# A scan-and-feed-forward kernel: ScalarE copies the first block's updates into the states instead of VectorE's additions

## The chip, the core and the metric

The kernel runs on one core of one Trainium2 chip. The metric is the device time of one execution in microseconds; the time of a kernel is the median of several executions. Engine names are those of the profile: PE is TensorE (its matmuls; PEld its weight loads), DVE is VectorE, ACT is ScalarE, POOL is GpSimd, SP is SyncE, which only issues transfers here.

## The reference

A gated linear attention over 768 positions is followed by two feed-forward layers over 3072 tokens of width 384, with 2048 hidden units each:

```
state = 0                                  # [4 batches, 8 heads, 48, 48]
for t in range(768):
    state = alpha[t][:, None] * state + outer(k[t], v[t])
    y[t]  = q[t] @ state
x = y as [3072 tokens, 384]
x = mish(x @ w_in) @ w_out                 # mish(h) = h * tanh(softplus(h))
out = (x' @ w2_in) -> h ; (h * cos(h)) @ w2_out
```

All of it is float32.

## The kernel before, in words

**The attention in chunks.** The sequence is cut into 6 blocks of 128 positions. A chunk c is one block of one batch: c = 4 * block + batch, so there are 24 chunks, and chunks 0 to 3 are the first block. For each chunk, a scan over the decays (`shrink`, line 713, into `suffix`) gives what is left of each key at the end of the chunk, and a second scan (`grow`, line 724, into `growth`) scales the queries. The products keys by suffix (`keys`) and queries by growth (`queries`) are made by VectorE for the first chunks and by GpSimd (lines 929 and 936) from chunk 4 on. TensorE turns the scaled keys (`turn`, line 370), multiplies keys by queries (`scores`, lines 394 and 387), and VectorE multiplies the scores by a triangle of ones and zeros (`mask`, line 746 or 752, into `probs`). TensorE then multiplies `probs` by the values (`values`, lines 434 and 439), adds what the state gives (line 453), and forms the chunk's update of the state: keys by values, in PSUM.

**The state.** `state` in SBUF holds, for each of the 4 batches, 4 pairs of heads, 96 rows (48 for each head of a pair, at partitions 0 and 64) and 96 columns. Only the blocks where a head meets itself may be non-zero; ScalarE sets the whole buffer to zero at the start (line 681, semaphore `state_zero`). The four updates of the first block lie in PSUM banks 3 and 4, two in each. `add_state(c)` (line 787) adds update c to the zeroed state of its batch, in two instructions of 48x192, one for each head of the pairs. Each counts up `sum_ready`. From chunk 4 on GpSimd first decays the state (`decay_state`, line 943, which wants `sum_ready` at 2 for chunk 4), and the two halves of a chunk are added by `add_first` (line 769) and `add_second` (line 778).

**The feed-forward layers in tiles.** 16 pieces of the weights and 6 blocks of tokens give 96 tiles per layer. A step s issues the first product of tile s (`first_product`, line 496, 9 matmuls of 128x512) and the second product of tile s - 3 (`second_product`, line 519, also 9). Float32 is split into a high and a low part: ScalarE makes the high part of a weight piece (line 573), and VectorE or GpSimd subtracts it from the raw piece to get the low part (`split_w`: line 800 on VectorE for pieces 1 and 3 of the first layer, line 914 on GpSimd for pieces 0, 2 and 4 to 15). ScalarE computes mish (line 619) and the high part of its result (line 612), GpSimd the low part (`g_rest`, line 922).

**The order around the change.** Each engine has one list of work written out by hand and runs it in that order; semaphores tie the lists together. TensorE runs chunks 0 to 3, then steps 0, 1, 2 ... In step 2 it also does `turn(4)` and `scores(4)`; in step 3 the first product of tile 3, then the update of chunk 4 (`halves_update`, line 413), `values(4)` and the second product of tile 0; in step 5 `turn(5)` and `scores(5)`; in step 7 `turn(6)`, the update of chunk 5, `scores(6)`, `values(5)`. `halves_update(4)` waits for the masks of chunk 4 (`probs_ready`), for all eight additions to the states (`sum_ready`) and for the turned keys; tile 3's first product waits for piece 3's low part from VectorE; `scores(c)` waits for the keys and queries of chunk c, and `scores(5)` for `add_second(4)` too. VectorE's list reads: low part of piece 1, `shrink(4)`, `grow(4)`, `add_state(0)`, low part of piece 3; then in step 1 `clear_probs` (line 759, which zeroes a quarter of `probs`) and `add_state(1)` to `add_state(3)`; in step 2 the masks of chunk 4; in step 3 `add_first(4)`, `shrink(5)`, `grow(5)`, `keep_x_lo(4)` (line 793), `add_second(4)`; in step 4 `shrink(6)`, `grow(6)`; in step 5 the masks of chunk 5. GpSimd's list reads: `keys(4)`, `queries(4)`, `decay_state(4)`, then low parts of mish and of weights in turn (tile 0, piece 4, tile 1, piece 5, tile 2, piece 6), `keys(5)`, `queries(5)`, `decay_state(5)`, tile 3, piece 7, `keys(6)`, `queries(6)`. ScalarE ends its start with the high part of piece 3 and goes on with mish of tile 0.

Of the kernel before, what the change touches and what calls it, by code (L numbers as in the profile page):

```python
# [8 lines left out]
ALU = mybir.AluOpType  # L9
ACT = mybir.ActivationFunctionType  # L10

BATCH, HEADS, SEQ, D = 4, 8, 768, 48
# [4 lines left out]
PAIRS = HEADS // 2  # L17
# [25 lines left out]
def values_at(s):  # L43

    n = s + FT - 3
    if s >= 3 and n % PER_CHUNK == 0 and n // PER_CHUNK < CHUNKS:
        return n // PER_CHUNK
    return None


def scores_at(s):

    return {2: BATCH, 5: BATCH + 1}.get(s)
# [54 lines left out]
def program(nc, aqk_in, v_in, w_in, mid, out):  # L108
    with ExitStack() as ctx:
        def sb(name, shape, dt=F32):  # L110
            return ctx.enter_context(nc.sbuf_tensor(name, shape, dt))

        def sem(name):
            return ctx.enter_context(nc.semaphore(name))
# [29 lines left out]
        state = sb("state", [P, BATCH, PAIRS, 2 * D])  # L144
# [42 lines left out]
        def update_of(c, half=None):  # L187

            if c < BATCH:
                return banks[3 + c // 2][:, c % 2 * PAIRS * D:(c % 2 + 1) * PAIRS * D]  # L190
            return (banks[1][:, 0:PAIRS * D], banks[6][:, P * 2:P * 2 + PAIRS * D])[half]
# [6 lines left out]
        state_zero = sem("state_zero")  # L198
# [18 lines left out]
        upd_done = sem("upd_done")  # L217
        sum_ready = sem("sum_ready")
# [22 lines left out]
        def alive(tile):  # L241
            return 0 <= tile < 2 * TILES
# [325 lines left out]
        def _(act):  # L568
            def split_w(piece):
                act.wait_ge(w_in_sem[piece % RAWS], 16 * (piece // RAWS + 1))  # L570
                if piece >= FT:
                    act.wait_ge(out_done, TILES - FT + piece - FT + 1)
                nc.scalar.activation(w_hi[:, piece % FT, :], w_raw[:, piece % RAWS, :], ACT.Copy).then_inc(whi_ready, 1)  # L573
# [8 lines left out]
            def keep_x_hi(c):  # L582
                j, b = c // BATCH, c % BATCH
                act.wait_ge(y_done, c + 1)
                if j >= 2 and b == 0:
                    act.wait_ge(h_done, FT * (j - 1))
                nc.scalar.activation(x_hi[:, j % 2, :, b * P:(b + 1) * P],
                                     turn_bank(c)[:, 0:DM].rearrange("p (k t) -> p k t", k=KT),
                                     ACT.Copy).then_inc(xhi_ready, 1)

            def split_x2(j, k):
                if k == 0:
                    act.wait_ge(x2_in, 16 * (j - BLOCKS + 1))
                    act.wait_ge(h_done, FT * (j - 1))
                nc.scalar.activation(x_hi[:, j % 2, k, :], x_raw[:, k, :], ACT.Copy).then_inc(xhi_ready, 1)
# [45 lines left out]
            def step(s):  # L641
                if alive(s - 1) and s - 1 < TILES:
                    g_part(s - 1)
                c = values_at(s)
                if c is not None and c > BATCH:
                    if next_scores(c) is not None:
                        keep_keys(next_scores(c))
                    keep_x_hi(c)
                if alive(s):
                    if s < TILES:  # L650
                        mish(s)
                    else:
                        turns(s)
                if s == 2 * TILES:
                    fold(s - 1)
                if alive(s - 2) and s - 2 >= TILES:
                    g_part(s - 2)
                if alive(s - 1) and s - 1 >= TILES:
                    if s < 2 * TILES:
                        fold(s - 1)  # L660
                    cosine(s - 1)
                if s % FT == LAG - 1 and s > FT:
                    take_acc(s // FT - 1)
                piece = split_at(s)
                if piece is not None:
                    split_w(piece)
                if scores_at(s) is not None:
                    keep_keys(scores_at(s))
                if values_at(s) == BATCH:
                    keep_x_hi(BATCH)  # L670
                jk = x2_split(s)
                if jk is not None:
                    split_x2(*jk)
# [24 lines left out]
            split_w(2)  # L698
            keep_x_hi(3)
            split_w(3)  # L700
            for s in range(STEPS):
                step(s)

        @block.vector
        def _(dve):
# [50 lines left out]
            def clear_probs():  # L756

                dve.wait_ge(y_done, BATCH)
                nc.vector.memset(probs[0:HALF, :, :, HALF:P], 0.0).then_inc(probs_zero, 1)
# [18 lines left out]
                    nc.vector.tensor_tensor(state[rows, c % BATCH, :, cols], update_of(c, 1)[rows, :].rearrange(  # L778
                        "d (p e) -> d p e", p=PAIRS), mid_state[rows, :, cols], ALU.add).then_inc(sum_ready, 1)

            def add_state(c):
                dve.wait_ge(upd_done, BATCH)
                dve.wait_ge(state_zero, 1)
                for i in range(2):
                    rows = slice(64 * i, 64 * i + D)
                    here = state[rows, c % BATCH, :, D * i:D * i + D]
                    nc.vector.tensor_tensor(here, update_of(c)[rows, :].rearrange("d (p e) -> d p e", p=PAIRS),
                                            here, ALU.add).then_inc(sum_ready, 1)

            def keep_x_lo(c):  # L790
                j, b = c // BATCH, c % BATCH
                dve.wait_ge(xhi_ready, c + 1)
                nc.vector.tensor_tensor(x_lo[:, j % 2, :, b * P:(b + 1) * P],
                                        turn_bank(c)[:, 0:DM].rearrange("p (k t) -> p k t", k=KT),
                                        x_hi[:, j % 2, :, b * P:(b + 1) * P].bitcast(F32),
                                        ALU.subtract).then_inc(xlo_ready, 1)

            def split_w(piece):
                dve.wait_ge(whi_ready, piece + 1)
                nc.vector.tensor_tensor(w_lo[:, piece % FT, :], w_raw[:, piece % RAWS, :],  # L800
                                        w_hi[:, piece % FT, :].bitcast(F32),
                                        ALU.subtract).then_inc(wlo_ready[1], 1)
# [15 lines left out]
            def reduce_angle(tile):  # L818
                n = tile - TILES
                part = banks[7]  # L820
                un, tn, h = u[:, tile % 2, :], t[:, tile % 3, :], h_of(tile)
                dve.wait_ge(u_ready, n + 1)
                nc.vector.tensor_scalar(un, un, ROUND, ROUND, ALU.add, ALU.subtract).then_inc(um_ready, 1)  # L823
                dve.wait_ge(um_ready, n + 1)
                nc.vector.scalar_tensor_tensor(part, un, -C1, h, ALU.mult, ALU.add).then_inc(rr_ready, 1)
                dve.wait_ge(rr_ready, n + 1)
                nc.vector.scalar_tensor_tensor(tn, un, -C2, part, ALU.mult, ALU.add).then_inc(w_ready, 1)  # L827
# [8 lines left out]
            def step(s):  # L836
                if alive(s) and s >= TILES:
                    reduce_angle(s)
                if alive(s - 1) and s - 1 >= TILES:
                    gate(s - 1)  # L840
                if s % FT == LAG - 1 and s > FT:
                    take_acc(s // FT - 1)
                if s == 1:
                    clear_probs()
                    for c in range(1, BATCH):
                        add_state(c)
                if scores_at(s) is not None:
                    mask(scores_at(s))
                c = values_at(s)
                if c is not None:  # L850
                    add_first(c)
                    if c == BATCH:
                        shrink(c + 1)
                        grow(c + 1)
                    keep_x_lo(c)
                    if next_scores(c) is not None:
                        mask(next_scores(c))
                    if c < UPDATES:
                        add_second(c)
                piece = split_at(s)  # L860
                if piece is not None and lo_owner(piece) == 1:
                    split_w(piece)
                c = prepared_at(s)
                if c is not None and c > BATCH + 1:
                    shrink(c)
                    grow(c)
                jk = x2_split(s)
                if jk is not None:
                    split_x2(*jk)
# [32 lines left out]
            split_w(1)  # L902
            shrink(4)
            grow(4)
            add_state(0)
            split_w(3)
            for s in range(STEPS):
                step(s)

# [118 lines left out]
```

## Time and profile before

| | us |
|---|---|
| median of 3 executions | 888.18 |
| the three executions | 887.71, 888.18, 893.39 |
| the profiled execution, device time | 889.28 |
| its span in the profile | 887.5 |
| TensorE busy | 876.0 (99%) |
| VectorE, ScalarE, GpSimd busy | 418.4, 411.1, 372.2 |
| mean granted TensorE clock | 0.998 of full |

The span is the time from the first to the last instruction that the profile shows; the device time of the same execution holds 1.78 us more. The rest of the document names times from the start of the span. A row such as "[0.96 <-DVE w_lo L800]" says that the engine sat idle for 0.96 us before the instruction, until VectorE's instruction of line 800 was done.

### The profile page before, as it was taken

The numbers are of one execution on the slowest core, as the hardware profiler recorded it, in microseconds if no ns is written. First come the engines' busy times: TensorE is split into PE (matmuls) and PEld (weight loads), VectorE is DVE, ScalarE is ACT, GpSimd is POOL, SyncE is SP. The second block draws the span as 40 slices with busy tenths as digits, with TensorE's granted clock in tenths as the row PEclk, the third lists the DMA queues.
The fourth block names the chain that finished last, engine by engine and source line by source line (L and its number), as shares of the span: only waits on it lengthen the run. The fifth ranks groups of instructions, "written<-read, shape, count | busy, mean of one in ns | idle before, by whom it ended". The sixth has DMA issues, their size and how long they took to land.

```text
span 887.5 us, 16403 instructions
## 1 busy us (share of the span) xinstructions
PE 876.0 (99%) x6686; PEld 727.4 (82%) x6686; DVE 418.4 (47%) x660; ACT 411.1 (46%) x707; POOL 372.2 (42%) x287
## 2 busy tenths in 40 slices
PE   8899999999999999999999999999999999999998
PEld 7688888888888888888888788888888888888886
DVE  8864322233332222230022766666565666666564
ACT  4444332232333233322455756565565656565554
POOL 3788654444345443432355433323232333323232
PEclk9999999999999999999999999999999999999999
DMA  9635321113212111210133200200200200200000
GB/s 223 191 105 150 88 75 39 40 41 87 64 44 75 39 41 40 75 31 1 54 124 108 72 1 1 71 1 1 72 0 1 72 1 0 72 1 1 37 0 36
DMA packets 17163, 48.28 MB, mean 54 GB/s; under 512 B 2752, under 2 KB 2752, under 8 KB 17088
## 3 DMA queue, kind: packets, MB, share of 16 engines
q1 hardware_dynamic: 17088, 47.23, 18.4%
q8 instruction: 53, 0.87, 0.4%
q14 instruction: 22, 0.18, 0.1%
HBM read 37.79 MB, written 9.44 MB: 53 GB/s over the span
## 4 chain that ended last, share of the span: by engine, by line
PE 94%; DVE 3%; issue 1%; ACT 1%; DMA 0%; POOL 0%; ACTq 0%; DVEq 0%; POOLq 0%
PE low L519 44%; PE low L496 33%; PE pair L496 11%; PE top L453 2%; PE top L434 1%; PE top L439 1%; PE pair L387 1%; PE low L413 1%; PE low L370 1%; DVE growth L724 1%; DVE suffix L713 0%; DMA shared<-aqk_in 0%; DVE w_lo L800 0%; DVE probs L746 0%; ACT w_hi L573 0%
## 5 line engine op out<-in xcount | busy, mean ns | idle before, releaser
L922 POOL TENSOR_TENSOR g_lo<-g,g_hi 128x512 fp32r<-128x512 f32 x192 | 260.9, 1359 | 471.2 <-ACT g_hi L612 471.2
L519 PE MATMUL low<-g_hi,w_hi 128*128 128x512 f32 x576 | 224.6, 390 | 0.3 <-DVE x_out L816 0.3
L519 PE MATMUL low<-g_hi,w_lo 128*128 128x512 f32 x576 | 224.1, 389 | 0.0
L612 ACT ACTIVATE g_hi<-g 128x512 fp32r<-128x512 f32 x192 | 120.6, 628 | 117.7 <-PE low L519 116.9
L519 PE MATMUL low<-g_lo,w_hi 128*128 128x512 f32 x576 | 165.7, 389 | 0.0
L519 PEld LDWEIGHTS low<-g_hi,w_hi 128*128 128x128 f32 x576 | 108.1, 188 | 23.8 <-DVE x_out L816 0.7
L519 PEld LDWEIGHTS low<-g_lo,w_hi 128*128 128x128 f32 x576 | 108.1, 188 | 22.6
L519 PEld LDWEIGHTS low<-g_hi,w_lo 128*128 128x128 f32 x576 | 108.1, 188 | 22.4
L496 PE MATMUL low<-x_hi,w_hi 128*128 128x512 f32 x432 | 124.0, 395 | 1.4 <-DVE w_lo L800 1.0
L496 PE MATMUL low<-x_lo,w_hi 128*128 128x512 f32 x432 | 121.6, 390 | 0.0
L496 PE MATMUL low<-x_hi,w_lo 128*128 128x512 f32 x432 | 121.5, 390 | 0.0
L619 ACT ACTIVATE g<-low 128x512 f32<-128x512 f32 x96 | 57.5, 599 | 135.9 <-PE low L496 135.9
L823 DVE TENSOR_SCALAR shared<-shared 128x512 f32<-128x512 f32 x96 | 42.2, 440 | 138.1 <-ACT shared L626 138.1
L496 PEld LDWEIGHTS low<-x_hi,w_lo 128*128 128x128 f32 x432 | 81.1, 188 | 17.3
L496 PEld LDWEIGHTS low<-x_lo,w_hi 128*128 128x128 f32 x432 | 81.1, 188 | 17.1
L496 PEld LDWEIGHTS low<-x_hi,w_hi 128*128 128x128 f32 x432 | 79.4, 188 | 19.0 <-issue 1.6
L769 DVE TENSOR_TENSOR mid_state<-low,state 48x192 f32<-48x192 f32 x40 | 14.2, 355 | 164.6 <-PE pair L413 124.5
L827 DVE SCALAR_TENSOR_TENSOR shared<-shared,top 128x512 f32<-128x512 f32 x96 | 65.9, 686 | 3.3
L626 ACT ACTIVATE shared<-low 128x512 f32<-128x512 f32 x48 | 28.7, 598 | 79.8 <-PE low L496 79.8
L626 ACT ACTIVATE shared<-pair 128x512 f32<-128x512 f32 x48 | 28.7, 598 | 74.2 <-PE pair L496 74.2
L639 ACT ACTIVATE shared<-shared 128x512 f32<-128x512 f32 x96 | 60.8, 633 | 3.0
L633 ACT ACTIVATE shared<-shared 128x512 f32<-128x512 f32 x96 | 59.8, 623 | 0.2 <-DVE shared L827 0.2
(107 smaller groups left out, 924.3 us busy)
## 6 DMA issues: line engine op xcount, KB each, us to landing
w_raw<-w_in SPq DMA_DIRECT2D x32, 384.0 KB, 3.1
shared<-aqk_in SPq DMA_DIRECT2D x44, 192.0 KB, 3.7
v_sb<-v_in SPq DMA_DIRECT2D x24, 256.0 KB, 4.4
shared<-aqk_in SPq DMA_DIRECT2D x48, 96.8 KB, 3.8
mid<-x_out SPq DMA_DIRECT2D x6, 768.0 KB, 5.3
shared<-mid SPq DMA_DIRECT2D x6, 768.0 KB, 5.8
out<-x_out SPq DMA_DIRECT2D x5, 768.0 KB, 4.1
out<-x_out SPq DMA_DIRECT2D x3, 256.0 KB, 2.4
```

The costliest lines, as they stand in the source:

```text
L453: mm = nc.tensor.matmul(turn[32 * n:32 * n + 32, k * P + t:k * P + t + HALF], ahead[0:ROWS, p, cols], q_of(c)[0:ROWS, p, t:t + HALF], star ...
L496: mm = nc.tensor.matmul(bank, wp[:, f, k * P:(k + 1) * P], xp[:, j % 2, k, :], start=(n == 0), stop=(n == 3 * KT - 1))
L519: mm = nc.tensor.matmul(acc[m], wp[:, f, DM + m * P:DM + (m + 1) * P], gp[:, tile % GB, :], start=(f == 0 and n == 0), stop=(f == FT - 1 a ...
L612: nc.scalar.activation(g_hi[:, tile % GB, :], g[:, tile % GB, :], ACT.Copy).then_inc(ghi_ready, 1)
L619: nc.scalar.activation(g[:, tile % GB, :], h_of(tile), ACT.Mish).then_inc(g_ready, 1)
L626: nc.scalar.activation(u[:, tile % 2, :], h_of(tile), ACT.Identity, scale=1.0 / TWO_PI).then_inc(u_ready, 1)
L633: nc.scalar.activation(here, here, ACT.Abs).then_inc(abs_ready, 1)
L639: nc.scalar.activation(here, here, ACT.Sin, scale=-1.0, bias=TWO_PI / 4).then_inc(r_ready, 1)
L769: nc.vector.tensor_tensor(mid_state[rows, :, cols], update_of(c, 0)[rows, :].rearrange("d (p e) -> d p e", p=PAIRS), state[rows, c % BATCH ...
L823: nc.vector.tensor_scalar(un, un, ROUND, ROUND, ALU.add, ALU.subtract).then_inc(um_ready, 1)
L827: nc.vector.scalar_tensor_tensor(tn, un, -C2, part, ALU.mult, ALU.add).then_inc(w_ready, 1)
L922: nc.gpsimd.tensor_tensor(g_lo[:, tile % GB, :], g[:, tile % GB, :], g_hi[:, tile % GB, :].bitcast(F32), ALU.subtract).then_inc(glo_ready, 1)
```

## The change

ScalarE gets a function `start_state(c)`, called for the four batches at the end of its start, between the high part of piece 3 and step 0. It copies the update of batch c out of PSUM into the zeroed state, in two ACTIVATE instructions of 48x192, after the zeroing of the state is done and after both updates of the PSUM bank are there. VectorE's `add_state` is gone, both the call for batch 0 before the low part of piece 3 and the three calls in step 1. `clear_probs` moves from step 1 to the place behind the low part of piece 3. The counts of `sum_ready` are the same.

```diff
--- before
+++ after
@@ scalar
+            def start_state(c):
+
+                act.wait_ge(state_zero, 1)
+                act.wait_ge(upd_done, c // 2 * 2 + 2)
+                for i in range(2):
+                    rows = slice(64 * i, 64 * i + D)
+                    nc.scalar.activation(state[rows, c, :, D * i:D * i + D], update_of(c)[rows, :].rearrange(
+                        "d (p e) -> d p e", p=PAIRS), ACT.Copy).then_inc(sum_ready, 1)
+
...
             split_w(2)
             keep_x_hi(3)
             split_w(3)
+            for c in range(BATCH):
+                start_state(c)
             for s in range(STEPS):
                 step(s)
@@ vector
-            def add_state(c):
-                dve.wait_ge(upd_done, BATCH)
-                dve.wait_ge(state_zero, 1)
-                for i in range(2):
-                    rows = slice(64 * i, 64 * i + D)
-                    here = state[rows, c % BATCH, :, D * i:D * i + D]
-                    nc.vector.tensor_tensor(here, update_of(c)[rows, :].rearrange("d (p e) -> d p e", p=PAIRS),
-                                            here, ALU.add).then_inc(sum_ready, 1)
...
-                if s == 1:
-                    clear_probs()
-                    for c in range(1, BATCH):
-                        add_state(c)
                 if scores_at(s) is not None:
                     mask(scores_at(s))
...
             shrink(4)
             grow(4)
-            add_state(0)
             split_w(3)
+            clear_probs()
             for s in range(STEPS):
                 step(s)
```

## Rows read from the trace of the kernel before

**Rows 1.** The page, busy time of each engine, its share of the span and instructions.

```profile
PE 876.0 (99%) x6686; PEld 727.4 (82%) x6686; DVE 418.4 (47%) x660; ACT 411.1 (46%) x707; POOL 372.2 (42%) x287
```

**Rows 2.** Waits of TensorE from 40 us on: us in total, times, longest.

```profile
PE low L413 <- DVE probs L752: 2.0, 1, 2.0
...
PE low L519 <- DVE x_out L816: 0.3, 1, 0.3
```

**Rows 3.** Timeline of TensorE: start us, us, what [idle before, releaser].

```profile
34.08 0.69 PE L387 MATMUL pair<-shared 48*64 48x64 f32 x32
...
35.73 0.94 PE L496 MATMUL low<-x_hi,w_hi 128*128 128x512 f32 x3 [0.96 <-DVE w_lo L800]
...
40.03 0.25 PE L413 MATMUL low<-v_sb,kd_t 64*48 64x48 f32 x2 [1.99 <-DVE probs L752]
...
43.76 0.50 PE L519 MATMUL low<-g_hi,w_hi 128*128 128x512 f32 x1
```

**Rows 4.** Windows: each engine's busy us, TensorE's granted clock, DMA share, GB/s.

```profile
40.03:43.83 3.80, 3.80 (x113) 3.41 (x113) 3.03 (x3) 0.00 (x0) 3.80 (x3) 0.55 0.50 151
...
59.90:62.64 2.74, 2.74 (x146) 2.58 (x145) 0.71 (x2) 0.84 (x2) 2.74 (x3) 1.00 0.16 33
```

**Rows 5.** Timeline of VectorE from 30 to 74 us.

```profile
30.47 2.17 DVE L724 TENSOR_TENSOR_SCAN growth<-shared,first_inv 112x516 f32<-112x516 f32 x1
...
33.32 2.27 DVE L800 TENSOR_TENSOR w_lo<-w_raw,w_hi 128x768 fp32r<-128x768 f32 x1
...
35.64 0.48 DVE L759 MEMSET probs<- 64x512 f32 x1
...
36.15 2.29 DVE L787 TENSOR_TENSOR state<-low,state 48x192 f32<-48x192 f32 x6
...
38.47 1.41 DVE L752 TENSOR_TENSOR probs<-pair,causal 64x512 f32<-64x512 f32 x2
...
41.51 4.12 DVE L713 TENSOR_TENSOR_SCAN suffix<-shared,first_one 112x516 f32<-112x516 f32 x1
...
55.27 1.41 DVE L752 TENSOR_TENSOR probs<-pair,causal 64x512 f32<-64x512 f32 x2
...
70.80 2.58 DVE L724 TENSOR_TENSOR_SCAN growth<-shared,first_inv 112x516 f32<-112x516 f32 x1
```

**Rows 6.** Line 800 on VectorE, durations in ns, min/median/max.

```profile
L800 DVE TENSOR_TENSOR w_lo<-w_raw,w_hi x10: 947/958/2268, 27.2 to 504.3; 128x768 fp32r<-128x768 f32 x10
```

**Rows 7.** Timeline of GpSimd from 32 to 75 us.

```profile
32.79 1.19 POOL L936 TENSOR_TENSOR shared<-shared,growth 112x512 f32<-112x512 f32 x1 [1.23 <-DVE growth L724]
...
33.93 0.83 POOL L943 TENSOR_TENSOR state<-state,suffix 112x384 f32<-112x384 f32 x1
...
41.48 1.27 POOL L922 TENSOR_TENSOR g_lo<-g,g_hi 128x512 fp32r<-128x512 f32 x1
...
48.19 1.19 POOL L936 TENSOR_TENSOR shared<-shared,growth 112x512 f32<-112x512 f32 x1 [1.23 <-DVE growth L724]
...
56.18 1.19 POOL L936 TENSOR_TENSOR shared<-shared,growth 112x512 f32<-112x512 f32 x1
...
72.25 2.12 POOL L929 TENSOR_TENSOR shared<-shared,suffix 112x512 f32<-112x512 f32 x1
```

**Rows 8.** Timeline of ScalarE from 26 to 33 us.

```profile
26.24 0.48 ACT L587 ACTIVATE x_hi<-low 128x384 fp32r<-128x384 f32 x1
...
29.15 0.60 ACT L619 ACTIVATE g<-low 128x512 f32<-128x512 f32 x1 [1.69 <-PE low L496]
...
31.57 0.60 ACT L619 ACTIVATE g<-low 128x512 f32<-128x512 f32 x1 [1.16 <-PE low L496]
```

**Rows 9.** Timeline of TensorE around the scores of chunks 5 and 6.

```profile
52.54 0.69 PE L387 MATMUL pair<-shared 48*64 48x64 f32 x32
...
59.90 0.25 PE L413 MATMUL low<-v_sb,kd_t 64*48 64x48 f32 x2
...
60.29 0.66 PE L387 MATMUL pair<-shared 48*64 48x64 f32 x32
```

## The prediction

> **What bounds the kernel now.** The page comes first: PE is busy for 99% of the span [rows 1], so only time in which PE waits, or runs at a lower clock, can be won. The view of waits says how much: from 40 us to the end PE waits once for 2.0 us and once for 0.3 us [rows 2]. The 2.0 us, and one wait of 0.96 us just before it, are the ones that this change touches. In PE's timeline the first product of tile 3 starts at 35.73 after 0.96 us of idling for piece 3's low part, and the update of chunk 4 starts at 40.03 after 1.99 us of idling for the masks [rows 3]. Behind the second wait the clock falls: in the 3.80 us of the update and values of chunk 4 the granted clock is 0.55 of full on average, so part of it ran at 1.2 GHz, while the same work of chunk 5, with 0.66 us of scores in it, takes 2.74 us at 1.00 [rows 4]. So the masks' delay costs its 1.99 us and a slow stretch. Everything after 43.8 us follows PE: what is won ahead of it is kept, unless another wait opens.
>
> VectorE's timeline shows why both are late [rows 5]: grow(4) ends at 32.64, then an addition to the state, piece 3's low part (2.27 us), the memset, six more additions (2.29 us), and only then, at 38.47, the masks, although the scores were done at 34.77 [rows 3].
>
> **A lock between VectorE and GpSimd.** Piece 3's low part took 2.27 us where the same line takes 0.95 undisturbed [rows 6]. Meanwhile GpSimd ran queries(4) until 33.98 and decay_state(4) until 34.76, both at their usual length [rows 7]. A real length of 0.86 us behind that gives the end at 35.59, so the two engines ran one after the other. shrink(5) shows it more strongly: 4.12 us from 41.51, beside GpSimd's work, for a scan that alone takes some 1.2. The additions and masks, which read PSUM, keep their lengths beside GpSimd (0.7 us a mask both in step 2 and in step 5). The Trainium skill has this as a rule (SBUF — State Buffer, "SBUF: two separate sides"): a VectorE instruction with two SBUF inputs and a GpSimd instruction exclude each other for the whole instruction, and the one that starts first has the port.
>
> **The change, part by part.** *Piece 3's low part.* VectorE issues it at about 32.6, ahead of queries(4), which start at 32.79 [rows 5, 7]; alone it takes 0.95 us and ends at 33.5. queries(4) then run from 33.5 to 34.7. That moves the scores of chunk 4 from 34.08 to 34.8; they take 0.69, so tile 3's first product starts at 35.5 and not 35.73: 0.2 us won, not 0.96. Were GpSimd first, the low part would end at 35.6 as now; the masks would still be in time, and the 0.2 us would be missing.
>
> *Masks.* The memset (0.48 us) is done at 34.0. The two masks (1.41 us) follow the scores from 35.5 to 36.9, under tile 3's product, which takes 2.3 us as now (from 35.73 to 40.03 less 1.99) and ends at 37.8. The 1.99 us are gone. With the 0.2 this is 2.2 us.
>
> *Clock.* PE then idles only 0.7 us or so ahead of the scores and not at all ahead of the update; the 0.96 us in the trace of before was followed by no slow stretch. At full clock the update and values take 2.74 - 0.66 = 2.1 us in place of 3.80: 1.7 us. Tile 0's second product starts at 39.8 instead of 43.8: about 4.0 us ahead, before what follows takes some back. add_first(4), two additions of 0.35 us, fits as it does in chunk 5 today.
>
> *ScalarE.* Eight copies of 48x192 out of PSUM are new. None of this shape exists. From above, a copy of 128x384 out of PSUM takes 0.48, the next starts 0.37 after it [rows 8]; eight by 0.48 are 3.9 us. From below, at half of the 0.37 us start-to-start, they are 1.5. I take 0.25 each, 2.0 us, since fewer elements are read but a fixed part stays. ScalarE now idles 1.69 us before mish of tile 0 at 29.15 and 1.16 us before the next at 31.57, so 2.0 us move the first mish by 0.3 and the second not at all. With 3.9 us tile 2's first product, which waits for that first mish, starts some 0.6 us late, and then the scores, which wait for queries(4) until 34.7 anyway, take it up. So its cost is zero over the whole range. The Trainium skill speaks against such small instructions (VectorE: DVE Perf Modes, the section on the TRN2 errata): its ScalarE line gives 172 + 192 cycles at 1.2 GHz, 0.30 us each; by that the estimate would be 2.4 us, and the time the same. The eight additions removed, six of which take 2.29 us [rows 5], free VectorE only; they touched no lock. The updates are complete before 27.46 (29.15 less 1.69), when ScalarE reaches them: tile 0's first product, behind them in PE's list, takes some 2.3 us and is done by 29.15, so it began before 26.9. No transfer is issued by the moved steps; load_w(7), which waits for piece 3's low part, comes 2 us earlier.
>
> *What is late next.* GpSimd. Its work from queries(4) on is contiguous but for two gaps of 1.23 us in which VectorE's scans hold the port [rows 7], so the chain of locked work from 32.6 to queries(5) and queries(6) has the same sum as before, only in another order. queries(5) now end at 48.19 + 1.19 = 49.4, and PE wants them at 52.54 [rows 9] less 4.0 = 48.5: a stall of 0.9 us, which leaves 3.1. queries(6) end at 56.18 + 1.19 = 57.4, and PE wants them at 60.29: of the gain at most 60.29 - 57.5 = 2.8 us is kept. The masks of chunk 5 end at 56.7 and PE wants them at 59.90, which allows 3.2. Beyond that I find no slack under 4 us: TensorE never waited for GpSimd afterwards, and GpSimd's next waits are for ScalarE, which follows TensorE. So **the sum is 2.8 us**. Against the profiled execution's own 889.28 this is 886.5; that execution lay 1.1 us above the median, so against the median of 888.18 it is 885.4.
>
> **The rivals.** *First come, first served at the port.* Because VectorE reaches shrink(5), grow(5) and shrink(6) about 3 us earlier, one more scan (1.2 us) could slip ahead of queries(5). For it: grow(7), asked for at 70.80, ran ahead of keys(7), which then took 2.12 us [rows 5, 7]. (The rule of the Trainium skill on the port, read as an order of arrival, would give this too.) Against it: shrink(5), asked for at 41.51, waited for the g_lo that had begun at 41.48 and for another GpSimd instruction behind it; GpSimd's instructions that had long been ready went first. Then queries(5) end at 50.5, PE stalls 2.0 us at scores(5), and 2.0 us are left: 886.2. A stall as long as today's 1.99 may bring the clock down again, another 1.7: 0.3 left, 887.9.
>
> *No later limit.* If the chain shortens, because a scan no longer makes GpSimd idle and overlaps better than I take, the whole 4.0 us stays: 884.2. Against it is shrink(5)'s 4.12.
>
> *Slower than before.* Both shrink(6) and grow(6) go ahead of queries(5), at 2.4 us together: queries(5) end at 51.8, PE stalls 3.3 us, 0.7 us of the 4.0 are left, and the clock falls behind it for 1.7: 1.0 us slower, 889.2. It decides whether the decays of chunk 6 have landed and shrink(6) is asked for before keys(5) begin, at about 47 us. Today VectorE reaches shrink(6) after 49; the load behind it waits for GpSimd's piece 5.
>
> *The change doesn't do what it says.* If the masks still hold PE, because something else in VectorE's list delays them, no more than 1 us is won: 887.5. Nothing in the rows points to it; the masks have 0.9 us of room.
>
> **How the numbers follow.** Forecast 0.52; first come first served 0.24, half of it with the lower clock; no later limit 0.12; slower 0.06; no effect 0.06. The predicted time is 885.4. The range reaches from 883.9 (no later limit, less 0.3 for the scatter between medians) to 888.0 (first come with the lower clock), and leaves out the slower case and part of the tails. A difference of 1%, 8.9 us, is about what a measurement can tell from no change; even the whole 4.0 us is 0.45%. All cases lie within it: faster by over 1% 0.02, within 1% 0.97, slower 0.01.
>
> **What would show it.** In the profile after: no wait of line 413 for line 752; clock at 1.00 from 37 to 44 us; tile 0's second product near 39.8; eight ScalarE copies of 0.25 to 0.35 us from 27.4; piece 3's low part near 0.95 us and queries(4) recorded longer; a new wait of PE for line 936 at line 387, about 0.9 us for chunk 5, and 0 to 0.3 for chunk 6; no waits after 60 us. I am wrong if PE waits over 1.5 us at scores(5) or at a clock below 1.00 there, or if tile 0's second product starts after 41.

## The result, and the profile after

The changed kernel takes 885.65 us (median of 16 executions, 885.27 to 887.33). The kernel before, measured beside it, takes 889.04 (median of 16, 887.43 to 893.39). The ratio is 0.9961, with a 95% interval from 0.9949 to 0.9973: 3.4 us less, between 2.4 and 4.5. The forecast was 2.8 us less, 885.4 us. The kernel before had shown 888.18 as the median of three; over 16 executions it is 0.9 us more, because five of the 16 took 890.7 us and more. Without these five the median is 888.67 and the difference 3.0 us. What makes an execution so long is likely to belong to this case (below).

The profiled execution of the changed kernel took 885.33 us, its span is 883.6 against 887.5. The page of the changed kernel, its busy times:

```profile
PE 874.8 (99%) x6686; PEld 726.4 (82%) x6686; DVE 417.1 (47%) x652; ACT 413.6 (47%) x715; POOL 372.7 (42%) x287
```

PE's waits in the changed kernel from 27 us to the end (us in total, times, longest), against [rows 2]:

```profile
PE pair L387 <- issue: 0.7, 1, 0.7
...
PE low L519 <- DVE x_out L818: 0.3, 1, 0.3
```

The 2.0 us for the masks is gone and so is the 0.96 us for piece 3's low part. A wait of 0.7 us at line 387, the scores of chunk 4, is new; the profile names no releaser for it ("issue"), but the scores start 0.10 us after queries(4) end (34.27, below).

The two executions are shifted against each other by 0.27 us from the start: grow(4) starts at 30.47 before [rows 5] and at 30.20 after. The differences below have this taken off. PE's timeline of the changed kernel (start, duration, what), against [rows 3] and [rows 9]:

```profile
34.37 0.69 PE L387 MATMUL pair<-shared 48*64 48x64 f32 x32 [0.67 <-issue]
...
35.00 0.96 PE L496 MATMUL low<-x_hi,w_hi 128*128 128x512 f32 x3
...
37.27 0.25 PE L413 MATMUL low<-v_sb,kd_t 64*48 64x48 f32 x2
...
39.46 0.50 PE L519 MATMUL low<-g_hi,w_hi 128*128 128x512 f32 x1
...
48.46 0.69 PE L387 MATMUL pair<-shared 48*64 48x64 f32 x32
...
56.47 0.69 PE L387 MATMUL pair<-shared 48*64 48x64 f32 x32
...
58.77 0.96 PE L496 MATMUL low<-x_hi,w_hi 128*128 128x512 f32 x3
```

One difference after the other. Tile 3's first product: 35.73 to 35.00, 0.46 us ahead. The update of chunk 4: 40.03 to 37.27, 2.49 ahead. Tile 0's second product: 43.76 to 39.46, 4.03 ahead. Scores of chunk 5: 52.54 to 48.46, 3.81 ahead. Scores of chunk 6: 60.29 to 56.47, 3.55 ahead. From there to the end nothing more is lost.

The window of the update and values of chunk 4 (busy us of each engine, then granted clock, DMA share, GB/s), against [rows 4]:

```profile
37.27:39.46 2.19, 2.19 (x113) 2.04 (x112) 1.48 (x3) 1.33 (x2) 2.19 (x3) 1.00 0.26 49
```

The same 113 matmuls took 3.80 us at 0.55 before and take 2.19 at 1.00. From the start of the update to tile 0's second product it is 3.73 us before and 2.19 after.

VectorE's timeline of the changed kernel, against [rows 5]:

```profile
30.20 2.18 DVE L735 TENSOR_TENSOR_SCAN growth<-shared,first_inv 112x516 f32<-112x516 f32 x1
...
32.30 0.93 DVE L802 TENSOR_TENSOR w_lo<-w_raw,w_hi 128x768 fp32r<-128x768 f32 x1
...
33.28 0.48 DVE L770 MEMSET probs<- 64x512 f32 x1
...
35.19 1.41 DVE L763 TENSOR_TENSOR probs<-pair,causal 64x512 f32<-64x512 f32 x2 [1.43 <-PE pair L387]
...
38.69 4.80 DVE L724 TENSOR_TENSOR_SCAN suffix<-shared,first_one 112x516 f32<-112x516 f32 x1
...
43.74 2.48 DVE L735 TENSOR_TENSOR_SCAN growth<-shared,first_inv 112x516 f32<-112x516 f32 x1
...
47.49 4.01 DVE L724 TENSOR_TENSOR_SCAN suffix<-shared,first_one 112x516 f32<-112x516 f32 x1
```

Piece 3's low part takes 0.93 us and not 2.27, because it is first at the port (the access to SBUF from which, as the prediction says, VectorE and GpSimd shut each other out). The masks run as soon as the scores are there. shrink(5), at 38.69, takes longer still than before, 4.80 us for a scan of 1.2; the last row is shrink(6).

GpSimd's timeline, against [rows 7]:

```profile
32.52 1.75 POOL L934 TENSOR_TENSOR shared<-shared,growth 112x512 f32<-112x512 f32 x1 [1.24 <-DVE growth L735]
...
42.37 2.77 POOL L912 TENSOR_TENSOR w_lo<-w_raw,w_hi 128x768 fp32r<-128x768 f32 x1
...
45.09 2.12 POOL L927 TENSOR_TENSOR shared<-shared,suffix 112x512 f32<-112x512 f32 x1
...
47.18 1.18 POOL L934 TENSOR_TENSOR shared<-shared,growth 112x512 f32<-112x512 f32 x1
...
55.18 1.18 POOL L934 TENSOR_TENSOR shared<-shared,growth 112x512 f32<-112x512 f32 x1
```

queries(4) take 1.75 us instead of 1.19: they wait for piece 3's low part. The next two rows are piece 6's low part and keys(5), with 2.77 and 2.12 us where 1.83 and 1.18 are usual. Each is a scan of VectorE that went ahead, and each costs GpSimd 0.94 us. Before, each of these scans cost GpSimd an idle gap of 1.23 us and more [rows 7], because GpSimd sat waiting for the scan's result. So queries(5) end at 48.36 and queries(6) at 56.36, both some 0.75 us earlier than before (with the shift).

ScalarE's timeline, against [rows 8]:

```profile
27.07 2.77 ACT L597 ACTIVATE state<-low 48x192 f32<-48x192 f32 x8
...
29.86 0.60 ACT L628 ACTIVATE g<-low 128x512 f32<-128x512 f32 x1
...
31.31 0.60 ACT L628 ACTIVATE g<-low 128x512 f32<-128x512 f32 x1 [0.19 <-PE low L496]
```

Eight copies take 2.77 us together, 0.35 each from start to start. The first mish follows without a gap and is 0.98 us later than before (29.15 to 29.86, with the shift); the second starts when PE releases it, as before.

### The profile page after: what moved, and what is told of

Same layout as the page of the kernel before. It is cut to its first block, busy times and chain, and to the rows that moved or that the text cites. A ratio compares the mean times of both kernels' runs of the same rounds, so it can differ in the third digit from the quotient of the medians.

```text
span 883.6 us, 16403 instructions
## 1 busy us (share of the span) xinstructions
PE 874.8 (99%) x6686; PEld 726.4 (82%) x6686; DVE 417.1 (47%) x652; ACT 413.6 (47%) x715; POOL 372.7 (42%) x287
## 4 chain that ended last, share of the span: by engine, by line
PE 95%; DVE 2%; ACT 1%; issue 1%; DMA 0%; POOL 0%; ACTq 0%; DVEq 0%; POOLq 0%
PE low L519 44%; PE low L496 34%; PE pair L496 11%; PE top L453 2%; PE top L434 1%; PE pair L387 1%; PE top L439 1%; PE low L413 1%; PE low L370 1%; DVE growth L735 1%; DVE suffix L724 0%; DMA shared<-aqk_in 0%; DVE probs L757 0%; ACT w_hi L573 0%; PE pair L413 0%
```

## The experiments

All kernels were timed in five rounds beside the kernel before, whose median was 888.66, 888.98 and 888.90 in the three sets, against 889.04 beside the changed kernel. The changed kernel was not timed again; its 885.65 is the value to compare with. The executions of one kernel fall into groups: eleven of the changed kernel took 885.3 to 886.1 us and five 886.7 to 887.3, all at a mean granted clock of 0.999 to 1.000. This step of some 1.3 us, which is not the clock, recurs in others (idle1, pe_order, pool_first, both_fence), so that a median can lie in either group. For differences smaller than that the profile decides; its measure is the start of tile 7's first product after the start of grow(4), 28.57 us in the changed kernel (58.77 less 30.20).

**Is the lower clock a part of it?** The first two put the idling back. `idle2`, and `idle1` with `range(3)`:

```diff
+                if s == 2:
+                    dve.wait_ge(scores_done, 2 * BATCH + 2)
+                    for i in range(5):
+                        nc.vector.memset(w_lo[0:HALF, FT - 1 - i, 0:512].bitcast(F32), 0.0)
                 if scores_at(s) is not None:
                     mask(scores_at(s))
```

> The changed kernel with five memsets of 64x512 (0.48 us each, into a part of w_lo that is written again later) put ahead of the masks of chunk 4, behind the scores. They push the end of the masks from 36.6 to about 39.2, so TensorE, ready for the update at 37.3, idles 2.0 us as in the kernel before. Clock theory (the 1.99 us of idling also cost a slow stretch of 1.7 us): granted clock well below 1.00 for some 3 us behind the wait, 2.0 + 1.7 us lost less up to 0.4 us that TensorE would have waited for GpSimd later, so 3.3 us above the changed kernel, about the kernel before. Rival (the idling counts alone, the slow stretch had another cause): clock at 1.00, 1.6 to 2.0 us above the changed kernel.

Measured: 888.51 us (887.04 to 889.93). PE's wait and the window behind it:

```profile
PE low L413 <- DVE probs L763: 2.0, 1, 2.0
...
39.79:43.51 3.72, 3.72 (x112) 3.33 (x113) 2.97 (x3) 0.00 (x0) 3.72 (x3) 0.54 0.47 129
```

> The same with three memsets: masks end at about 38.2, TensorE idles 1.0 us. Clock theory and rival agree that the clock stays at 1.00 if a wait of 1 us is short enough: 0.6 to 1.0 us above the changed kernel. If the clock falls here too, some 2.5 us above it.

Measured: 886.91 us (885.84 to 887.67).

```profile
PE low L413 <- DVE probs L763: 0.9, 1, 0.9
...
38.36:40.62 2.26, 2.19 (x113) 2.08 (x113) 1.50 (x3) 0.53 (x1) 2.26 (x2) 1.00 0.53 151
```

With 2.0 us of idling the update and values of chunk 4 take 3.72 us at a clock of 0.54; with 0.9 us they take 2.26 at 1.00. idle2's median is 2.9 us above the changed kernel, tile 7's first product comes 3.08 us later in its profile (3.3 expected), and the slow stretch is there again: in this execution the clock theory holds. idle1's median is 1.3 us above, more than the 0.6 to 1.0 expected, but its lowest time is 0.57 above and tile 7's product 0.47 later; the rest is the step between the groups. The slow stretch does not come in every execution. Of the twelve of idle2, eight took 888.3 to 889.9, at a mean granted clock of 0.997 to 0.999; four took 887.0 to 887.5 at 0.999 to 1.000, and the lowest of them is 1.8 us above the lowest of the changed kernel, which fits the idling alone. These groups can't be put down to the clock as a whole, since the step of 1.3 us is mixed in. The kernel before has 31 of its 105 executions at 887.1 to 887.9, which would fit no slow stretch; no trace of one was taken.

**Must the additions leave VectorE, or only come later?** `late_adds`: no copies on ScalarE, the additions moved.

```diff
             grow(4)
             split_w(3)
+            add_state(0)
...
                     mask(scores_at(s))
+                if s == 2:
+                    for c in range(1, BATCH):
+                        add_state(c)
```

> VectorE keeps the eight additions, ScalarE copies nothing; the additions only move: batch 0's behind piece 3's low part, the other six behind the masks of chunk 4. Theory (what ends last ahead of the update decides, and the work must leave VectorE): masks end at 36.6, the additions at about 38.9, TensorE idles 1.7 us for line sum_ready in place of the masks; 1.3 to 1.7 us above the changed kernel without a fall of the clock, 3.0 to 3.4 with one. Rival (the order on VectorE is what was wrong, the engine doesn't matter): within 0.3 us of the changed kernel.

Measured: 887.28 us (886.80 to 889.72), 1.6 above the changed kernel.

```profile
PE low L413 <- DVE state L796: 1.9, 1, 1.9
...
39.40:41.64 2.24, 2.19 (x113) 2.08 (x113) 1.49 (x3) 0.00 (x0) 2.24 (x3) 1.00 0.57 183
```

The wait has changed its name: 1.9 us for line 796, the additions, and not for the masks. So moving them back within VectorE's list, to these places, isn't enough. Other places were not tried. VectorE sits idle for 1.43 us ahead of the masks in the changed kernel and for 0.7 us between the masks and the start of the update, 2.1 us together, and eight additions take 3.1 (six took 2.29 [rows 5]): by this estimate any order leaves PE waiting for about 1 us. In this execution 1.9 us of idling left the clock at 1.00; nine of the twelve took under 888.

**What does the port do if GpSimd is first?** `queries_first`:

```diff
             grow(4)
+            dve.wait_ge(qd_ready, BATCH + 1)
             split_w(3)
```

> The changed kernel, but VectorE waits for queries(4) before it makes piece 3's low part, so that GpSimd has the port first. Theory (the two exclude each other, either order has the same sum): queries(4) end about 0.55 us earlier, the scores of chunk 4 start at 33.8, piece 3's low part ends at 35.1 (after queries(4) or after decay_state(4)), tile 3's first product starts at 35.1 to 35.5 against 35.0: 0 to 0.3 us above the changed kernel. Rival (the 0.67 us idle ahead of the scores is not caused by the port): queries(4) unchanged, tile 3's product late by the whole wait, 0.7 us or more above.

Measured: 888.05 us (886.54 to 889.26), 2.4 above the changed kernel and 1.3 between the lowest times, where the theory had 0 to 0.3. The rival's 0.7 or more came true as a number, but not its reason: queries(4) take 1.19 us and not 1.75, so it was the port that held them in the changed kernel. The rows are piece 3's low part on VectorE, then queries(4), decay_state(4) and tile 0's low part on GpSimd, then tile 3's first product on PE:

```profile
33.96 2.80 DVE L802 TENSOR_TENSOR w_lo<-w_raw,w_hi 128x768 fp32r<-128x768 f32 x1 [1.37 <-POOL shared L935]
...
32.73 1.19 POOL L935 TENSOR_TENSOR shared<-shared,growth 112x512 f32<-112x512 f32 x1 [1.23 <-DVE growth L735]
...
33.89 0.83 POOL L942 TENSOR_TENSOR state<-state,suffix 112x384 f32<-112x384 f32 x1
...
34.68 1.26 POOL L921 TENSOR_TENSOR g_lo<-g,g_hi 128x512 fp32r<-128x512 f32 x1
...
35.91 2.54 POOL L913 TENSOR_TENSOR w_lo<-w_raw,w_hi 128x768 fp32r<-128x768 f32 x1
...
36.91 0.93 PE L496 MATMUL low<-x_hi,w_hi 128*128 128x512 f32 x3 [2.19 <-DVE w_lo L802]
```

Piece 3's low part was asked for at 33.96, 0.07 us behind decay_state(4). It got the port neither behind that nor late in tile 0's low part, but at 35.9, when both were done; the low part of piece 4, also ready, waited for it this time. PE idled 2.19 us, and from 36.91 to 40.90 the granted clock was 0.60. The sum of the work is the same, but the order in which it is served is not that of the asking.

`one_add` leaves one of the four additions where it was:

```diff
-            for c in range(BATCH):
+            for c in range(1, BATCH):
                 start_state(c)
...
             grow(4)
+            add_state(0)
             split_w(3)
```

(`add_state(0)` waits for ScalarE's copies of batch 1, which reads the same PSUM bank, and `decay_state` for all eight.)

> The changed kernel, but VectorE still makes batch 0's addition, ahead of piece 3's low part; ScalarE copies the other three. Theory (one addition of 0.7 us lets GpSimd's queries(4) have the port first, and decay_state(4) behind it): piece 3's low part ends at 35.3 to 35.6 instead of 33.2, tile 3's first product starts 0.4 to 0.5 us later than in the changed kernel; the masks are still in time; 0.2 to 0.5 us above the changed kernel. Rival (piece 3's low part has slack, and nearly all of the gain is the six additions): under 0.1 us.

Measured: 885.72 us, but from 885.57 to 893.76. Eight executions took 885.6 to 885.8, 0.3 above the lowest of the changed kernel; two took 893.1 and 893.8. The profiled one is the former of these two. Piece 3's low part, GpSimd's instructions beside it, and tile 3's first product:

```profile
33.27 8.23 DVE L812 TENSOR_TENSOR w_lo<-w_raw,w_hi 128x768 fp32r<-128x768 f32 x1
...
33.89 0.84 POOL L952 TENSOR_TENSOR state<-state,suffix 112x384 f32<-112x384 f32 x1
...
34.68 1.27 POOL L931 TENSOR_TENSOR g_lo<-g,g_hi 128x512 fp32r<-128x512 f32 x1
...
35.91 1.81 POOL L923 TENSOR_TENSOR w_lo<-w_raw,w_hi 128x768 fp32r<-128x768 f32 x1
...
37.66 1.27 POOL L931 TENSOR_TENSOR g_lo<-g,g_hi 128x512 fp32r<-128x512 f32 x1
...
38.88 1.81 POOL L923 TENSOR_TENSOR w_lo<-w_raw,w_hi 128x768 fp32r<-128x768 f32 x1
...
40.64 2.00 POOL L931 TENSOR_TENSOR g_lo<-g,g_hi 128x512 fp32r<-128x512 f32 x1
...
41.65 1.62 PE L496 MATMUL low<-x_hi,w_hi 128*128 128x512 f32 x3 [6.92 <-DVE w_lo L812]
```

This is the surprise of the study. VectorE asked for the port at 33.27 and was done at 41.50, 8.23 us for an instruction that alone takes 0.93. Meanwhile GpSimd ran five instructions at their usual length, one behind the other without a gap; VectorE came in ahead of the sixth, which was ready too. PE idled 6.92 us. One addition of 0.71 us ahead of piece 3's low part is enough to let queries(4) have the port first, and then it is open when VectorE gets it: behind decay_state(4), as in the trace of before, or, as here, behind queries(4) and five more.

**Does that explain the kernel before?** It has the same addition in the same place, and 35 of its 105 executions in this study took 890 us or more: 15 of them 890.2 to 891.8, and 20 of them 893.3 to 895.4. The 96 executions of the eight kernels in whose profile VectorE has the port first (the changed kernel, idle2, idle1, late_adds, and below pe_order, pool_first, both, both_fence) stay under 890, every one. `before_fence`, an edit of the kernel before, makes GpSimd stop once:

```diff
                 pool.wait_ge(ghi_ready, tile + 1)
+                if tile == 0:
+                    pool.wait_ge(wlo_ready[1], 2)
```

> The kernel before with one wait added: GpSimd begins the low part of mish of tile 0 only when VectorE has made piece 3's low part. One order of the work, which the trace of before shows, is left as it is; the other, in which GpSimd goes on through its ready instructions while VectorE waits for the port, is closed. Theory (those executions of the kernel before that take 890 us and more are such starved ones, as the one that the profile of one_add caught with 8.2 us for piece 3's low part): the lowest time stays at 887.3 to 887.6, none lies above 889.8, median 887.5 to 889. Rival (they have another cause): the spread up to 893 to 895 stays in about one execution of six.

Measured: 888.14 us (886.45 to 889.49). Not one of twelve is above 889.5, where six of the 23 executions of the kernel before beside it are above 890 (up to 894.25, median 888.90). Twelve without any would come by chance in 0.8% of cases at the share of all 105, one in three, and in 2.7% at the share of these 23. The lowest, 886.45, is below what was expected; in the profiled execution VectorE came in ahead of decay_state(4), which the wait also allows. The difference of the medians, 0.8 us, is not clear of noise (ratio 0.9993, 0.9981 to 1.0006).

So the order at the port is the likely cause of the long executions and not a shown one: no long execution of the kernel before has a trace, the two groups above 890 are not told apart, and queries_first, where GpSimd also has the port first, has none above 889.3 in twelve.

The same profile has a case against a simple reading of the clock. PE idled for the masks as long as in the trace of before, and the update and values behind it took 2.19 us at 1.00 (the wait, then the window):

```profile
39.23 0.25 PE L413 MATMUL low<-v_sb,kd_t 64*48 64x48 f32 x2 [1.98 <-DVE probs L752]
...
39.23:41.42 2.19, 2.19 (x112) 2.05 (x112) 1.49 (x3) 0.00 (x0) 2.19 (x2) 1.00 0.62 187
```

Over the profiles, the clock fell behind an idling of 1.99 us (before, idle2), 2.19 (queries_first) and 6.92 (one_add), and stayed at 1.00 behind 1.98 (before_fence), 1.9 (late_adds) and 0.9 (idle1). An idling of 1.9 to 2.0 us can bring it down, and doesn't always.

**Is GpSimd's chain what takes back 0.5 us?** `pe_order` takes away PE's 0.7 us at the scores of chunk 4; `pool_first` makes queries(5) and queries(6) earlier; `both` has both edits.

```diff
@@ tensor (pe_order)
                 if scores_at(s) is not None:
                     turn(scores_at(s))
-                    scores(scores_at(s))
-                if c == BATCH:
-                    halves_update(c)
-                    values(c)
+                    if s != 2:
+                        scores(scores_at(s))
+                if c == BATCH:
+                    scores(BATCH)
                 if alive(s - LAG):
                     second_product(s - LAG)
+                if c == BATCH:
+                    halves_update(c)
+                    values(c)
@@ gpsimd (pool_first)
+                c = prepared_at(s)
+                if c is not None and s < 5:
+                    prepare(c)
                 piece = split_at(s)
                 if piece is not None and lo_owner(piece) == 0:
                     split_w(piece)
-                c = prepared_at(s)
-                if c is not None:
+                if c is not None and s >= 5:
                     prepare(c)
```

> The changed kernel, but TensorE does tile 3's first product ahead of the scores of chunk 4, and tile 0's second product between those scores and the update, so that neither queries(4) (0.67 us idle) nor the masks are waited for. Forecast's theory (from here on GpSimd's chain up to queries(5) and queries(6) limits how far TensorE can be ahead): TensorE starts tile 4's first product 0.35 us earlier (tile 3's product can't start before mish of tile 2 is done at 34.0), but waits as much more for queries(5): the end moves by under 0.15 us. Rival (there is still room in the chain): 0.3 to 0.7 us below the changed kernel.

Measured: 885.99 us (885.18 to 886.95), no gain, as the forecast's theory had it. grow(4) on VectorE, then on PE tile 3's first product, the scores of chunk 5 and tile 7's first product:

```profile
30.20 2.18 DVE L738 TENSOR_TENSOR_SCAN growth<-shared,first_inv 112x516 f32<-112x516 f32 x1
...
34.01 0.96 PE L496 MATMUL low<-x_hi,w_hi 128*128 128x512 f32 x3 [0.30 <-ACT g L631]
...
48.46 0.69 PE L387 MATMUL pair<-shared 48*64 48x64 f32 x32 [0.30 <-issue]
...
58.76 0.98 PE L496 MATMUL low<-x_hi,w_hi 128*128 128x512 f32 x3
```

Tile 7's product comes 28.56 us after grow(4), against 28.57. What was gained ahead is waited for at the scores of chunk 5, 0.30 us.

> The changed kernel, but in steps 3 and 4 GpSimd makes keys, queries and decay of chunks 5 and 6 ahead of the low parts of weight pieces 6 and 7 instead of behind them. Theory (after the change TensorE's last short waits, 0.2 us ahead of scores(5) and 0.1 to 0.2 ahead of scores(6), are for queries(5) and queries(6)): queries(5) end 1 us or more earlier, both waits are gone, pieces 6 and 7 are still in time: 0.2 to 0.4 us below the changed kernel. Rival (they are something else, such as an instruction's issue): unchanged within 0.1 us in the profile's start of the second product behind scores(6).

Measured: 885.71 us (884.88 to 886.99). grow(4), queries(5) on GpSimd, tile 7's first product, and PE's longest wait:

```profile
30.34 2.18 DVE L735 TENSOR_TENSOR_SCAN growth<-shared,first_inv 112x516 f32<-112x516 f32 x1
...
45.50 1.21 POOL L934 TENSOR_TENSOR shared<-shared,growth 112x512 f32<-112x512 f32 x1
...
58.43 0.97 PE L496 MATMUL low<-x_hi,w_hi 128*128 128x512 f32 x3
...
PE top L453 <- issue: 1.3, 1, 1.3
```

queries(5) end at 46.71, 1.8 us earlier, and tile 7's product comes after 28.09 us: 0.48 less (0.2 to 0.4 expected), so the short waits were for queries(5) and queries(6). The median doesn't show it beside a scatter of 2 us. This execution then lost 1.3 us at 372 us of the span, where PE waited for nothing that the profile shows. Its time, 886.35, lies in the upper group of its kernel (six at 886.0 to 887.0, six at 884.9 to 885.4). The profile of before_fence lost 0.97 us at the same matmul, near 375 us. So a stall of this kind is likely to be the step between the groups.

> The edits of the two others together. If GpSimd's chain is what holds, freeing it lets TensorE keep what the other order gains: 0.6 to 0.8 us below the changed kernel, more than the two alone add up to. If it isn't, the sum of the two.

Measured: 885.00 us (median of 8, 884.65 to 886.14), 0.65 below the changed kernel.

```profile
30.46 2.18 DVE L738 TENSOR_TENSOR_SCAN growth<-shared,first_inv 112x516 f32<-112x516 f32 x1
...
58.39 0.97 PE L496 MATMUL low<-x_hi,w_hi 128*128 128x512 f32 x3
```

27.93 us, 0.64 less than the changed kernel. Alone, the order on PE gave 0.01; with the chain freed it adds 0.16. The chain was the limit, as the forecast had it.

**The best version** is `both` with the wait of before_fence added (`both_fence`):

> The version of both (ScalarE's copies, the other order on TensorE, keys and queries of chunks 5 and 6 first on GpSimd) with the same added wait. Piece 3's low part is already first at the port there, so the wait costs nothing and bars nothing: median 884.7 to 885.3, within 0.3 us of both, some 0.6 us below the changed kernel, and 4 us below the kernel before. If the wait's own cost shows (a late start of tile 0's low part), up to 0.3 us more.

Measured: 884.94 us (median of 12, 884.61 to 886.37), ratio to the kernel before 0.9947 (0.9927 to 0.9968). Tile 7's product comes after the same 27.93 us as in both, so the added wait cost nothing; it bars an order that did not occur there.

```profile
30.35 2.18 DVE L738 TENSOR_TENSOR_SCAN growth<-shared,first_inv 112x516 f32<-112x516 f32 x1
...
58.28 0.97 PE L496 MATMUL low<-x_hi,w_hi 128*128 128x512 f32 x3
```

## Why the prediction was right, step by step

**Piece 3's low part**: right in kind. VectorE was first at the port, 0.93 us (forecast 0.95), and queries(4) recorded longer. Tile 3's product was 0.46 us ahead and not 0.2: queries(4) lost 0.56 us, where 0.7 had been taken. The sentence that the other order at the port would only miss 0.2 us holds for eight of the twelve executions of one_add (0.3 us above the changed kernel, lowest against lowest) and fails for the others. It took for granted that VectorE gets the port after at most two of GpSimd's instructions. In queries_first it came later, and the median was 2.4 us higher, a fall of the clock included; one_add lost up to 8.

**Masks and clock**: right. 2.49 us ahead at the update (forecast 2.2), 4.03 at tile 0's second product (forecast 4.0); the clock's part is the difference, 1.54 (forecast 1.7). idle2 brings the slow stretch back by idling alone, idle1 with half the idling doesn't. Not foreseen was that 2.0 us of idling doesn't always do it (before_fence); where it doesn't, the change is worth less, perhaps the 2.2 us between the lowest times, 887.43 and 885.27.

**ScalarE**: no cost, as forecast. Its copies took 0.35 us each, not the 0.25 taken; 2.77 us together, inside the bounds of 1.5 and 3.9. The measured value lies above the 0.30 us estimated from the Trainium skill (VectorE: DVE Perf Modes, the section on the TRN2 errata) too, and that estimate came nearer than the forecast's. The first mish was 0.98 us later with no one behind it waiting.

**What is late next**: the mechanism right, the size wrong, and this is the mis-sized term. The forecast said that the chain of locked work up to queries(5) and queries(6) "has the same sum as before", and took back 0.9 us at the scores of chunk 5 and 1.2 in all, leaving 2.8. The chain became 0.75 us shorter: a scan that goes ahead while GpSimd has work costs GpSimd 0.94 us, one whose result GpSimd waits for costs 1.23; two scans make 0.58, and the rest stood before tile 0's low part. 0.48 us were taken back, and 3.55 stayed. pe_order, pool_first and both show that the chain is indeed the limit; the sum was off, not the place.

**The time**: that 885.4 came so near to 885.65 is in part luck. The gain was forecast 0.6 us too small (2.8 against 3.4 between the medians), and the median of three it was taken from, 888.18, lay 0.9 us under that of 16; the two cancel. The 3.4 us are also no pure measure of the mechanism: the long executions of the kernel before are in it, of which the forecast says nothing. The two profiles, one execution each, give the 3.55.

**The rivals.** First come, first served: no further scan went ahead of queries(5). shrink(6) was asked for at 47.49, 0.31 us after queries(5) had started, because shrink(5), asked for at 38.69, was itself passed over by two GpSimd instructions that started at 39.32 and 41.12. PE lost only 0.2 us at the scores of chunk 5. The Trainium skill's rule on the port (SBUF — State Buffer, "SBUF: two separate sides"), that the two exclude each other for a whole instruction, agrees with the rows shown here; read as an order of arrival it doesn't: in one_add an instruction asked for at 33.27 came behind five that started later. No later limit: its gain, 4.0 us, is nearer to the 3.55 of the profiles than the forecast's 2.8, its time, 884.2, is further from the measured one, and its mechanism is wrong, since the chain did take something back. The slower case didn't occur.

## What to carry to other kernels

Work on an engine with free time may still be what another waits for: the eight additions cost nothing by VectorE's share of busy time and over 2 us by their place in its list. When a wait is taken away, count what its idling did to TensorE's clock too, and look for the shared resource that will hold next. And where VectorE and GpSimd share the port, give a critical VectorE instruction with two SBUF inputs the first place (0.93 us in the changed kernel, 2.27 in the trace of before, 8.23 in one_add), or make GpSimd wait once for its result: the order between ready instructions isn't yours.

## What was not expected of the hardware

VectorE can be kept from the port through several ready instructions of GpSimd: 8.23 us in one_add, 4.80 for shrink(5) in the changed kernel. At other times it comes in between two ready instructions, as behind decay_state(4) in the trace of before. What decides it stays open. Nor is it settled why 1.99 us of idling brings the clock down in one execution and 1.98 in another doesn't, nor what the 1.3 us at 372 us in the profile of pool_first and the 0.97 us in that of before_fence are.
